# Opening of a fused attention and mixture-of-experts kernel: one load per head, and queries and keys turned and summed by fours in one product

## What is computed

```python
# q, k, v: 4 batches x 8 heads x 576 positions x 64
q_d = q.reshape(B, H, S // 4, 4, D).mean(axis=3)      # k_d, v_d alike
out_d = sm_attn(q_d, k_d, v_d)                        # pooled attention, 144 x 144
out_up = np.repeat(out_d, 4, axis=2)
mask = np.abs(pos[:, None] - pos[None, :]) < 4        # local attention
scores = np.where(mask, scale * q @ k.T, -1e9)
out_local = softmax(scores) @ v
x = out_up + out_local                                # 2304 rows x 512
x = _moe_ref(x, ...)      # 8 experts, 288 tokens each, assigned by a greedy order
return _moe2_ref(x, ...)  # 512 -> 2048 -> 512, a leaky unit with one slope per column
```

## Time and profile before

| | |
|---|---|
| median of 3 runs | 903.95 us (902.13 to 904.32) |
| the profiled execution, its own time | 905.23 us |
| its span | 903.5 us |
| mean granted PE clock | 0.969 of full |
| PE, DVE, ACT, POOL busy in the span | 94%, 70%, 35%, 16% |
| attention | from 0 to about 196 us |

### The profile page before, as it was taken

One profiled execution on the slowest core, in us unless ns is written; L12 is line 12 of the kernel. 1 busy time (PEld: TensorE's weight loads), 2 busy tenths in 40 slices (PEclk: granted clock), 3 DMA queues, 4 the chain that ended last, 5 costly groups with the idle time before them and its releaser, 6 DMA issues.

```text
span 903.5 us, 19231 instructions
## 1 busy us (share of the span) xinstructions
PE 849.1 (94%) x7220; PEld 756.0 (84%) x7220; DVE 636.1 (70%) x1715; ACT 319.5 (35%) x1009; POOL 145.4 (16%) x186
## 2 busy tenths in 40 slices
PE   7899999862899999999999999999999999999996
PEld 7577778651798899899889888998898899899995
DVE  4687879558889867876786567668767866875332
ACT  2566767632453341143134112421331242143111
POOL 4754646310000200110020001100200110010001
PEclk9899999985799999999999999999999999999998
DMA  7667561033652320430142021303400430340000
GB/s 163 150 151 193 132 164 51 16 96 111 202 181 87 116 90 2 125 118 1 57 124 67 1 85 50 116 1 95 126 22 1 142 101 1 94 152 1 1 1 35
DMA packets 122676, 77.27 MB, mean 86 GB/s; under 512 B 64280, under 2 KB 105240, under 8 KB 122584
## 3 DMA queue, kind: packets, MB, share of 16 engines
q1 hardware_dynamic: 119416, 65.83, 26.5%
q0 software_dynamic: 3168, 10.23, 3.7%
HBM read 66.59 MB, written 9.44 MB: 84 GB/s over the span
## 4 chain that ended last, share of the span: by engine, by line
PE 67%; DVE 9%; issue 2%; ACT 0%; POOL 0%; DVEq 0%; POOLq 0%; ACTq 0%
PE banks L967 21%; PE banks L968 19%; PE banks L969 19%; PE banks L988 2%; PE banks L972 2%; PE banks L973 1%; DVE neg L1364 1%; PE banks L976 1%; PE banks L1017 1%; DVE w1s L1444 1%; DVE wout L1444 1%; DVE onehot L1317 1%; DVE hid L1372 1%; DVE win L1444 1%; DVE act L1366 0%
## 5 line engine op out<-in xcount | busy, mean ns | idle before, releaser
L1546 ACT CAST hid<-act 128x256 fp32r<-128x256 f32 (+1 forms) x128 | 55.5, 434 | 335.8 <-DVE act L1366 328.1
L967 PE MATMUL banks<-xy,win 128*128 128x256 f32 (+1 forms) x448 | 136.2, 304 | 2.1 <-DVE act L1366 2.1
L969 PE MATMUL banks<-xy,win 128*128 128x256 f32 (+1 forms) x448 | 132.7, 296 | 0.0
L968 PE MATMUL banks<-xy,win 128*128 128x256 f32 (+1 forms) x448 | 132.6, 296 | 0.0
L1364 DVE TENSOR_SCALAR neg<-banks,alph 128x256 f32<-128x256 f32 (+1 forms) x128 | 66.1, 516 | 90.5 <-PE banks L969 76.3
L967 PE MATMUL banks<-wout,hid 128*128 128x512 f32 x288 | 117.0, 406 | 0.6 <-DVE hid L1372 0.4
L968 PE MATMUL banks<-wout,hid 128*128 128x512 f32 x288 | 113.5, 394 | 0.0
L969 PE MATMUL banks<-wout,hid 128*128 128x512 f32 x288 | 112.8, 392 | 0.0
L1581 POOL DMA_INDIRECT rows<-x_rows,id_new x24 | 23.7, 985 | 499.5 <-DVE id_new L1325 494.6
L561 ACT ACTIVATE prob<-banks,nbias 96x102 f32<-96x102 f32 (+1 forms) x256 | 85.9, 350 | 22.4 <-DVE nbias L474 12.6
L967 PEld LDWEIGHTS banks<-xy,win 128*128 128x128 f32 x448 | 85.4, 191 | 6.1 <-DVE act L1366 3.1
(11 more groups left out here) (216 smaller groups left out, 1863.1 us busy)
## 6 DMA issues: line engine op xcount, KB each, us to landing
raw<-in_moe_w SPq DMA_DIRECT2D x128, 256.0 KB, 3.6
qn<-in_q SPq DMA_DIRECT2D x48, 96.0 KB, 2.6
kn<-in_k SPq DMA_DIRECT2D x48, 96.0 KB, 2.5
vn<-in_v SPq DMA_DIRECT2D x8, 576.0 KB
x_rows<-xs SPq DMA_DIRECT2D x24, 192.0 KB, 2.1
raw<-in_moe_w_in SPq DMA_DIRECT2D x16, 256.0 KB, 3.5
raw<-in_moe_w_out SPq DMA_DIRECT2D x16, 256.0 KB, 3.4
vw<-in_v SPq DMA_DIRECT2D x16, 204.0 KB
```

Source lines behind the costliest of these rows:

```text
L967: nc.tensor.matmul(out_ap, a_hi, b_hi, start=start, stop=False)
L968: nc.tensor.matmul(out_ap, a_lo, b_hi, start=False, stop=False)
L969: return nc.tensor.matmul(out_ap, a_hi, b_lo, start=False, stop=stop)
L1546: nc.scalar.copy(hid[:, (FC + j) % 3, 0, 0:CHUNK[k]], act[:, j % 2, 0:CHUNK[k]]).then_inc(h_hi, 1)
```

## The change

1. Loads of queries and keys: one transfer per head with all six blocks (96 x 6 x 64), 16 per batch instead of 24. In batch 0 they are issued by pairs of heads, with a semaphore for the queries and one for the keys of each pair; the first half of v goes ahead of the fourth pair.
2. The window loads are cut in two: 96 rows, and the 6 (or 3) that are left, 12 transfers per batch instead of 6.
3. In batch 0 each block of 96 positions is multiplied with `turn_and_sum` (96 x 120: the identity, and beside it the 24 columns that sum fours) instead of being transposed. The bank then holds turned values and their sums; DVE or ACT copies the sums straight from the bank to `qdT` or `kdT` (`pool_first`) before it copies the turned values. The two reductions per pair are gone in batch 0.
4. The plan of the opening: one pair of heads per step instead of two pairs in the first; in steps up to 0 the maximum of the new item stands ahead of the normalization of the last one; the turned probabilities of item 0 stand ahead of the fourth pair; the second half of v is summed one step later.
5. The fills: 9 instead of 18 at the start, none before the units. The three products with ones stay ahead of the scores of items 4 and 5; those ahead of items 2 and 3 are left out.
6. POOL makes the tile of ones, then the masks, and then the constants of the expert stage.

```diff
         def qk(b, hp, units):
             self.steps += [("qk", b, (t, hp, c)) for t, c in units]
-            if units[-1] == (1, 1):
+            if b > 0 and units[-1] == (1, 1):
                 self.steps.append(("pool", b, hp))
...
         for t in range(-LAG, NU + 3):
             b, s = t // NI, t % NI
-            first = {-LAG: (0, 1), 1 - LAG: (2,), 2 - LAG: (3,)}.get(t, ())
-            for hp in first:
-                qk(0, hp, all_four)
+            if t == 0:
+                self.steps += [("flip", t, 0), ("flip", t, 1)]
+            if t + LAG < HP:
+                qk(0, t + LAG, all_four)
             if 0 <= t + LAG < NU:
                 self.steps.append(("scores", t + LAG, 0))
             if 0 <= t + LAG - 1 < NU:
                 self.steps.append(("exp", t + LAG - 1, 0))
-            if 0 <= t < NU:
+            if 0 < t < NU:
                 self.steps += [("flip", t, 0), ("flip", t, 1)]
+            if t <= 0:
+                self.steps.append(("max", t + LAG, 0))
             if 0 <= t + LAG - 1 < NU:
                 self.steps.append(("normalize", t + LAG - 1, 0))
-            if t in (1 - LAG, 2 - LAG):
-                self.steps += [("pool_v", 0, 3 * (t + LAG - 1) + stage) for stage in range(3)]
-            if 0 <= t + LAG < NU:
+            if t in (1 - LAG, 3 - LAG):
+                self.steps += [("pool_v", 0, 3 * (t + LAG - 1) // 2 + stage) for stage in range(3)]
+            if 0 < t and t + LAG < NU:
                 self.steps.append(("max", t + LAG, 0))
...
-        heads = slice(half * H // 2, (half + 1) * H // 2)
         for dst, src in ((qn, q), (kn, k)) if part is None else (((qn, q), (kn, k))[part],):
-            for r in range(R):
-                e.dma_start(dst[:, r, heads], src[b, heads, r * T:(r + 1) * T].rearrange("h p d -> p h d")
-                            ).then_inc(qk_in[half], 16)
+            for h in range(half * H // 2, (half + 1) * H // 2):
+                e.dma_start(dst[:, :, h], src[b, h].rearrange("(r p) d -> p r d", p=T)).then_inc(qk_in[half], 16)
+
+    def load_first_qk(e, hp):
+
+        for t, (dst, src) in enumerate(((qn, q), (kn, k))):
+            for h in range(2 * hp, 2 * hp + 2):
+                e.dma_start(dst[:, :, h], src[0, h].rearrange("(r p) d -> p r d", p=T)).then_inc(qk_first[t][hp], 16)
...
         for j in range(NT):
             lo, hi = (PAD if j == 0 else 0), (W - PAD if j == NT - 1 else W)
-            s0 = j * T - PAD + lo
-            e.dma_start(vw[lo:hi, b % 2, j, :].rearrange("p (h d) -> p h d", h=H),
-                        vt[b, s0:s0 + hi - lo]).then_inc(vw_in[b % 2], 16)
+            for a, z in ((lo, lo + T), (lo + T, hi)):
+                e.dma_start(vw[a:z, b % 2, j, :].rearrange("p (h d) -> p h d", h=H),
+                            vt[b, j * T - PAD + a:j * T - PAD + z]).then_inc(vw_in[b % 2], 16)
...
     def sync(e):
-        load_qk(e, 0, 0)
-        load_qk(e, 0, 1)
+        for hp in range(HP - 1):
+            load_first_qk(e, hp)
         load_v(e, 0, 0)
+        load_first_qk(e, HP - 1)
         load_v(e, 0, 1)
         e.wait_ge(pads_made, 4)
         load_windows(e, 0)
...
         t, hp, c = unit
-        if (t, c) == (0, 0) and hp % (HP // 2) == 0:
-            e.wait_ge(qk_in[hp // (HP // 2)], 16 * 2 * R * (b + 1))
+        if b == 0 and c == 0:
+            e.wait_ge(qk_first[t][hp], 16 * 2)
+        elif (t, c) == (0, 0) and hp % (HP // 2) == 0:
+            e.wait_ge(qk_in[hp // (HP // 2)], 16 * H * b)
         pe_bank_free(e, "qk", b, unit)
         bank = pF[PLAN.place["qk", b, unit] % RING]
-        if b == 0:
-            pe_fill(bank, 1)
+        if (b, unit) == (0, (0, 0, 0)):
+            e.wait_ge(fours_made, 2)
         for x in range(R // 2):
+            if b == 0:
+                last = nc.tensor.matmul(bank[:, x * FOURS:(x + 1) * FOURS],
+                                        (qn, kn)[t][:, c * (R // 2) + x, 2 * hp:2 * hp + 2, :].rearrange("p h d -> p (h d)"),
+                                        turn_and_sum[:], start=True, stop=True)
+                continue
             last = nc.tensor.transpose(bank[:, x * T:(x + 1) * T], (qn, kn)[t][:, c * (R // 2) + x, 2 * hp:2 * hp + 2, :].rearrange("p h d -> p (h d)"),
                                        ident[0:T, 0:T])
         last.then_inc(flipped, 1)
...
         if u == 0:
-            e.wait_ge(consts["fixed_made"], consts["ones_at"])
-        if 2 <= u <= LAG + 2:
+            e.wait_ge(consts["ones_made"], 1)
+        if HP <= u <= LAG + 2:
             pe_dense(psum[:, 512 * 7:512 * 8], 3)
         if u >= 2:
             e.wait_ge(exped, u - 1)
         if kind == "pooled":
-            e.wait_ge(pooled_qk, b * HP + x + 1)
+            e.wait_ge(pooled_qk, (b + 1) * HP + x + 1 if b else 2 * (x + 1))
...
             if x == 0:
-                e.wait_ge(pooled_qk, b * HP + HP)
+                e.wait_ge(pooled_qk, (b + 2) * HP)
             if u == HP:
+                for c in range(2):
+                    wait_emptied(e, "qk", 0, (1, HP - 1, c))
                 e.wait_ge(masks_made, 1)
...
     def tensor(e):
         e.wait_ge(consts["made"], consts["n_made"])
-        pe_fill(pF[0], 18)
+        pe_fill(pF[0], 9)
...
+        if b == 0:
+            return engine_copy(dst[:, c * (S // 2):(c + 1) * (S // 2)].rearrange("p (x n) -> p x n", n=T), first_bank(unit)[:, :, 0:T],
+                               SCALE if t == 0 else None)
         return engine_copy(dst[:, c * (S // 2):(c + 1) * (S // 2)], pF[PLAN.place["qk", b, unit] % RING][:, 0:S // 2],
                            SCALE if t == 0 else None)
...
+    def first_bank(unit):
+        return pF[PLAN.place["qk", 0, unit] % RING][:, 0:R // 2 * FOURS].rearrange("p (x n) -> p x n", n=FOURS)
+
+    def pool_first(e, engine_copy, unit):
+
+        t, hp, c = unit
+        e.wait_ge(flipped, PLAN.flipped("qk", 0, unit))
+        part = (qdT, kdT)[t][:, 0, hp, c * HALF:(c + 1) * HALF].rearrange("p (x n) -> p x n", n=T // FACTOR)
+        copied = engine_copy(part, first_bank(unit)[:, :, T:FOURS], SCALE if t == 0 else None)
+        if t == 1:
+            copied.then_inc(pooled_qk, 1)
...
     def vector(e):
+        e.wait_ge(consts["made"], 2)
+        nc.vector.tensor_copy(turn_and_sum[:, 0:T], ident[0:T, 0:T]).then_inc(fours_made, 1)
+        nc.vector.tensor_reduce(turn_and_sum[:, T:FOURS], ident[0:T, 0:T].rearrange("p (m r) -> p m r", r=FACTOR), AX.X, ALU.add
+                                ).then_inc(fours_made, 1)
         nc.vector.memset(kT[:, :, :, 0:PAD], 0.0).then_inc(pads_made, 1)
         nc.vector.memset(kT[:, :, :, PAD + S:], 0.0).then_inc(pads_made, 1)
         nc.vector.memset(vw[:, :, 0, :], 0.0).then_inc(pads_made, 1)
...
         for kind, u, x in STEPS:
             if kind == "qk" and x[2] == 0:
+                if u == 0:
+                    pool_first(e, dve_copy, x)
                 empty_qk(e, dve_copy, u, x).then_inc(emptied_dve, 1)
             elif kind == "pool":
                 dve_pool(e, u, x)
@@ -569,6 +611,8 @@
         for kind, u, x in STEPS:
             pooled = kind == "apply" and ITEMS[u][0] == "pooled"
             if kind == "qk" and x[2] == 1:
+                if u == 0:
+                    pool_first(e, act_copy, x)
                 empty_qk(e, act_copy, u, x).then_inc(emptied_act, 1)
...
-    def gpsimd(e):
+    def gpsimd(e, make_fixed):
         band = consts["pool_steps"]
         m = mask[:].rearrange("p v h w -> p v h w")
         nc.gpsimd.memset(mask[:], 0.0).then_inc(band, 1)
@@ -633,6 +677,7 @@
                                         base=base, pattern=pattern, channel_multiplier=per_row).then_inc(band, 1)
                 e.wait_ge(band, at)
         nc.gpsimd.memset(consts["spare"][:], 0.0).then_inc(masks_made, 1)
+        make_fixed(e)
...
-    for t in ("ones", "segment", "before"):
+    n, tiles, at, cut_at = 7, NT * T // TILE // B, 0, 0
+
+    for t in ("segment", "before"):
...
-            make_route_consts(nc, e, fixed, T, NT, E, J, TILE, SLOTS, B, fixed_made)
-            attn["gpsimd"](e)
+            nc.gpsimd.memset(fixed["ones"][:], 1.0).then_inc(ones_made, 1)
+            attn["gpsimd"](e, lambda e: make_route_consts(nc, e, fixed, T, NT, E, J, TILE, SLOTS, B, fixed_made))
```

More of the change, by code:

```diff
@@ L154, in attention @@
     mask = sb("mask", [T, 3, 4, W], BF16)
+    FOURS = T + T // FACTOR
+    turn_and_sum = sb("turn_and_sum", [T, FOURS], F32)
     ident, ident16 = consts["ident"], consts["ident16"]
@@ L165, in attention @@
     qk_in = [sem("qk_in0"), sem("qk_in1")]
+    qk_first = [[sem(f"{t}_first{hp}") for hp in range(HP)] for t in "qk"]
+    fours_made = sem("fours_made")
     vn_in, wg_in = [sem("vn_in0"), sem("vn_in1")], sem("wg_in")
@@ L378, in pe_apply @@
             if x == 0:
-                e.wait_ge(vw_in[b % 2], 16 * NT * (b // 2 + 1))
+                e.wait_ge(vw_in[b % 2], 16 * 2 * NT * (b // 2 + 1))
             e.wait_ge(summed, b * NT + x)
@@ L678, in make_route_consts @@
```

(10 more changed lines are left out.)

## The result

The changed kernel takes 897.2 us (median of five runs; the four that agree lie between 896.21 and 897.42, one was disturbed), the kernel before 902.98 beside it. The ratio is 0.992, with an interval of 0.990 to 0.993: 6 to 9 us faster by the interval, 5.8 us by the two medians. Forecast were 899.0 us and a gain of 5.0.

The account below looks back on a forecast made before the run. The opening was taken as a serial chain through PE, DVE and ACT, with attention afterwards at PE's pace. A 5.0 us gain at the third local scores carries through: 903.95 - 5.0, rounded 899.0 us; range 894.0 to 902.5.

Parts of the forecast that it names:

- The chain to the first scores: Opening, from fills through units, table load and copies: first pooled scores start at 10.5 us instead of 15.26.
- The small pieces eat the gain: Rival: 128x72 copies cost 0.45 us and handoffs 0.2, losing some 3.5 us: 902.5 us; chance 0.15 together with slow windows.
- From pair to pair: Opening's serial chain: second to fourth pooled scores at 14.2, 18.2, 23.2 us, first local scores at 25.2 instead of 29.95.
- The next steps: Second and third local scores: 28.8 instead of 33.65 us and 32.8 instead of 37.87; gain there 5.0 us.
- What is hidden: Opening: dropped fills and ones save nothing; POOL's constants keep 3 us of cover, v's second half 1 us.
- SP and the loads: Cut windows let batch 1's loads start at 25.8 us; first half there by 35.3, ahead of use at 37.7.
- this case: Rival, windows stay slow: PE waits 3.2 us for batch 1's half, gain 1.8; chance 0.15 together with dear small pieces.
- The rival on the low stretch: Low clock from 38.2 to 48.4 us goes: 4 us more won, 895 us; chance 0.18.
- The slower rival: Clock sinks more in the opening, 8 to 33 us: 7.3 us lost against 5.0 won, 906.2 us; chance 0.07.

Follow-up runs that it names:

- the eleventh experiment: Changed kernel with early table load, four fills instead of nine, and batch 1's first queries and keys issued ahead of batch 0's windows: 914.47, 911.04, 913.66 and 896.55 us.
- the undisturbed trace of before: Second trace of the kernel before, nothing changed, no low clock between 20.4 and 48 us: 903.68 us, span 901.4.
- the first experiment: Changed kernel with v's window loads whole again, 6 transfers per batch instead of 12: 903.82 us, ratio 0.999 to the kernel before.
- block loads: Changed kernel with queries and keys of batches 1 to 3 loaded by blocks of 96 positions of four heads again: 897.71 us, ratio 0.992.
- table load ahead: Changed kernel with a one-column activation ahead of ACT's list, so that the table load runs earlier: 898.29 us, ratio 0.993.
- The four-fill kernel: Changed kernel with early table load and 4 fills instead of 9 at the start: median 908.98 us, profiled execution 899.28.
- the ninth experiment: Changed kernel with transposes and DVE reductions back in batch 0, and four fills instead of one ahead of each of its units: 915.04 us, ratio 1.013.

## Why the prediction was right

**The chain to the first scores.** Forecast 10.5, measured 10.19; the table load at 8.2, measured 8.10. Fills ended at 6.1 as worked out (first unit at 6.12). A unit costs 0.72 us at the high clock (10.83 to 12.27 for two), not 0.67, and 1.36 at the low one (11.25 to 13.96 for two in the kernel of the eleventh experiment); a 128x72 copy takes 0.23 us on DVE, where I took 0.2. "The small pieces eat the gain" falls with that.

**From pair to pair.** Forecast 14.2, 18.2, 23.2 and 25.2; measured 14.09, 18.09, 23.39 and 25.02.

**The next steps.** Forecast 28.8 and 32.8, measured 28.54 and 31.90. Here the sum was 0.9 us short: item 4's maximum was through earlier than I had it (ACT starts its exponentials at 29.14, PE's scores follow at 31.90). That is nearly all of the difference between 5.0 and the 5.7 against the undisturbed trace of before.

**What is hidden** stayed so. POOL's constants ended at 13.3, item 0 came to it at 16.26 (forecast 16.4), item 3's normalization ran from 30.51 to 31.8 (forecast 30.4 to 31.7).

**SP and the loads** was the step on which it all hung, and the first experiment shows it: with whole windows 903.8 us, where I had put this case at 902.2, with a wait of 3.2 us instead of 4.6 and without the low clock that came with it. SP came to batch 1's loads at 25.18 (forecast 25.8). But PE took its first unit at 34.75, 2.9 us earlier than my 37.7, and the last of its keys, issued at 29.38, landed 5.1 us later, at 34.5 (forecast 35.3): the cover I claimed, 2.4 us, is 0.3. The step at fault is the 42.68 from which I took 5.0: it lay inside the low stretch. In the second trace of the kernel before PE was there at 40.90 and already waited 0.16 us for these keys, and of two kernels with openings within 0.2 us of the changed one's, one waited 0.5 us for them (block loads) and one 0.2 (table load ahead, first unit at 35.15). The wait of 0.5 us cost nothing, since the changed kernel's PE waits 0.48 us for exponentials right behind this unit anyway (its next local scores start at 35.95, those with block loads at 35.92). So the real margin is a little under 0.8 us. That it was enough is in part luck: PE came 2.9 us earlier than I reckoned, against a cover of 2.4, and the landing happened to be 0.8 earlier too. The four-fill kernel, whose opening is 1.9 us faster, falls into just this wait.

**The rival on the low stretch** is half right. The stretch is absent in the changed kernel's trace, and in the first pair of traces the distance in attention is 8.3 us instead of 5.6 because of it; but the kernel before has executions without it. What brings it stays open: neither ones in the wait nor leaving them out in the changed kernel decided it. The traces, laid side by side, show this much: each stretch that the clock column shows at 0.50 in the first 60 us, in whatever kernel, began during a long wait of PE or at most 2 us behind one (waits of 1.19 and 1.30 us in the first trace of before, 1.28 in the second, 1.29 to 4.6 in the experiments). Other waits as long had none behind them (1.29 at 37.81 in the second trace of before, 2.12 at 12.55 in the kernel of the ninth experiment). In the changed kernel's trace no wait of the opening, once PE has begun, exceeds 0.84 us. That this is why it has no such stretch is likely, but not shown.

**The slower rival** did not happen, but the kernel of the eleventh experiment is its picture, and my price was too low. I priced one unit of each pair on the chain and 0.2 us for the scores (they cost 0.5: 1.24 against 0.71), 3.3 us to the first local scores. At the low clock all four units and the scores bound a pair (4 x 1.36 + 1.16 = 6.6 us of PE, measured 7.0), and the first local scores come at 34.88, 9.9 us after those of the changed kernel.

**How the parts share the gain**, in medians against the kernel before beside each: loads alone 2.6 us, loads and product (and fills, and POOL's order) 3.5, all with the plan 5.8. The first two can't be told apart (ratios of 0.996 for both, with intervals of 0.995 to 0.998), so in the old plan the product gains nothing measurable; the new plan without the product loses 4 us against before. With the new loads, product and plan gain only together. Everything without the cut windows gains nothing measurable. Fewer fills at the start and POOL's order were not tried by themselves, and no trace shows what the old number of fills would do in the changed kernel. No version beat the changed kernel.

## What to carry to other kernels

When an opening is made faster, work out when the next batch's first data is used and when it lands: here a change of 5 to 6 us rested on a margin of less than 1 us, bought by cutting six transfers so that their main part has 96 rows. A new order of steps is worth only as much as the work that fills it: the same plan won 2 to 3 us with one product per block and, with fewer fills too, lost 7 with transposes and a separate sum. And before a difference between two traces is explained, take a second trace of the slower kernel: 3.5 of 9.4 us here belonged to one execution.

## What the runs showed of the hardware

- The number of fills at the start decides over 11 us. With the table load ahead and nine fills, five executions took 896.5 to 898.9 us; with four fills instead, seven of eight took 907.7 to 914.8 and one 899.3; with four fills and batch 1's loads ahead, three of four took 911.0 to 914.5 and one 896.6. The one profile of such a slow execution has the whole opening, to 38 us, at 1.2 GHz.
- PEclk reads 1.00 until the first change in the record, also where the same scores take 1.24 us instead of 0.71; in the opening the durations must be read.
- With 144 KB per transfer the DMA share exceeds 1 (1.16 at 198 GB/s in 25 to 38 us of the changed kernel; with 96 KB per transfer 0.78 at 171 in the same stretch, and 0.84 at 189 in the earlier trace rows), so it isn't a measure of fullness there; GB/s is.
- Windows of 102 or 99 rows load at 116 GB/s in a stretch nearly their own (first experiment, 47.9 to 58.0 us), the same bytes cut into 96 rows and a rest at 175 (changed kernel, 43.3 to 50.2 us).
